# Output products in 32-row bands, decays from logarithms and exponentials, all stacking issued from SP

## The reference

```python
mag = np.sqrt(a_re * a_re + a_im * a_im)
scale = np.minimum(mag, 0.999) / (mag + 1e-06)
a_re_n, a_im_n = (a_re * scale, a_im * scale)      # 4 batches, 8 heads, 768 steps, 48 wide
for t in range(S):
    new_re = ar * S_re - ai * S_im
    new_im = ar * S_im + ai * S_re
    S_re, S_im = (new_re + kv, new_im)              # kv = k_t outer v_t
    y[:, :, t] = np.einsum('bhd,bhde->bhe', q[:, :, t], S_re)
x = y as [3072 tokens, 384]
h = x @ w_in;  g = h * clip(h + 3, 0, 6) / 6;              x = g @ w_out      # 384 -> 2048 -> 384
h = x @ w_in;  g = max(h, 0) + alpha * min(h, 0);          out = g @ w_out
```

## Time and profile before

| | us |
|---|---|
| three runs | 1082.05, 1083.62, 1083.95 |
| median | 1083.62 |
| the profiled execution | 1083.26 |
| its span, first to last instruction | 1081.5 |
| PE busy | 1009.7 (93%) |
| DVE busy | 703.4 (65%) |
| ACT busy | 487.5 (45%) |
| POOL busy | 305.8 (28%) |

### The profile page before, as it was taken

How to read it: one execution, slowest core, us unless ns; L and a number is a source line. 1 busy time by engine, 2 the same in 40 slices (tenths; PEclk the granted TensorE clock), 3 DMA queues, 4 the chain that set the end, 5 groups by cost and what they waited for, 6 DMA issues and landing times.

```text
span 1081.5 us, 16917 instructions
## 1 busy us (share of the span) xinstructions
PE 1009.7 (93%) x6354; PEld 1005.0 (93%) x6354; DVE 703.4 (65%) x1234; ACT 487.5 (45%) x814; POOL 305.8 (28%) x291
## 2 busy tenths in 40 slices
PE   0477789999999999999999999999999999999998
PEld 0477789999999999999999999999999999999997
DVE  4966999998998988889988234553433434343332
ACT  4644765676656666667664244331212212122221
POOL 3213421222222222222122233333333233333332
PEclk9968999999999999999999999999999999999999
DMA  5451233323233333232222070100101010101000
GB/s 182 132 147 30 67 95 99 94 67 88 68 77 102 87 87 89 67 89 67 70 74 74 13 277 1 45 24 22 45 1 44 1 45 1 44 1 45 1 22 23
DMA packets 77858, 70.47 MB, mean 65 GB/s; under 512 B 32592, under 2 KB 73552, under 8 KB 77392
## 3 DMA queue, kind: packets, MB, share of 16 engines
q1 hardware_dynamic: 68176, 61.07, 19.4%
q10 hardware_dynamic: 9600, 8.33, 2.9%
HBM read 40.90 MB, written 9.44 MB: 47 GB/s over the span
## 4 chain that ended last, share of the span: by engine, by line
PE 86%; DVE 7%; issue 2%; ACT 2%; SPq 1%; DMA 1%; ACTq 0%; DVEq 0%
PE op L995 12%; PE op L997 12%; PE op L996 12%; PE hp L997 12%; PE hp L995 12%; PE hp L996 12%; PE yp L980 5%; PE yp L983 4%; PE gp L990 2%; PE gp L959 2%; PE yp L959 2%; DVE t_inv L649 1%; PE tp L968 1%; DVE t_phase L665 1%; SPq L335 1%
## 5 line engine op out<-in xcount | busy, mean ns | idle before, releaser
L439 POOL TENSOR_TENSOR g_lo<-gated,g_hi 128x384 fp32r<-128x384 f32 x256 | 269.5, 1053 | 697.4 <-ACT g_hi L528 697.3
L528 ACT ACTIVATE g_hi<-gated 128x384 fp32r<-128x384 f32 x256 | 133.5, 522 | 357.5 <-DVE gated L761 291.4
L757 DVE TENSOR_SCALAR gate<-hp,alpha_sb 128x384 f32<-128x384 f32 x128 | 79.1, 618 | 230.5 <-PE hp L997 230.5
L995 PE MATMUL op<-g_hi,wb_hi 128*128 128x384 f32 x384 | 135.4, 353 | 2.3 <-POOL g_lo L439 2.3
L995 PE MATMUL hp<-x_hi,wa_hi 128*128 128x384 f32 x384 | 131.1, 341 | 6.1 <-DVE gated L747 6.1
L521 ACT ACTIVATE gate<-hp,half 128x384 f32<-128x384 f32 x128 | 73.7, 576 | 126.8 <-PE hp L997 115.0
L995 PE MATMUL op<-g_hi,wa_hi 128*128 128x384 f32 x384 | 129.9, 338 | 0.7 <-issue 0.7
L996 PE MATMUL op<-g_lo,wb_hi 128*128 128x384 f32 x384 | 130.0, 338 | 0.0
L997 PE MATMUL op<-g_hi,wb_lo 128*128 128x384 f32 x384 | 129.9, 338 | 0.0
L997 PE MATMUL op<-g_hi,wa_lo 128*128 128x384 f32 x384 | 129.8, 338 | 0.0
L997 PE MATMUL hp<-x_hi,w2i_lo 128*128 128x384 f32 x384 | 129.5, 337 | 0.0
(11 more groups left out here) (97 smaller groups left out, 1978.5 us busy)
## 6 DMA issues: line engine op xcount, KB each, us to landing
st<-prod SPq DMA_DIRECT2D x48, 145.1 KB, 3.1
st<-prod ACTq DMA_DIRECT2D x48, 145.1 KB, 2.8
a_sb<-a_in SPq DMA_DIRECT2D x24, 288.0 KB, 3.5
qk_sb<-qk_in SPq DMA_DIRECT2D x24, 288.0 KB, 3.5
v_pad<-v_in SPq DMA_DIRECT2D x24, 192.0 KB, 3.2
x<-out_sb SPq DMA_DIRECT2D x8, 576.0 KB, 2.8
x_raw<-x SPq DMA_DIRECT2D x8, 576.0 KB, 4.6
out<-out_sb SPq DMA_DIRECT2D x8, 576.0 KB, 3.1
```

Of the source, the lines that this page charges most:

```text
L439: pool.tensor_tensor(g_lo[:, at, :], gated[:, at * UT:(at + 1) * UT], g_hi[:, at, :].bitcast(F32), ALU.subtract).then_inc(glo_done, 1)
L528: act.activation(g_hi[:, at, :], gated[:, at * UT:(at + 1) * UT], ACT.Copy).then_inc(ghi_done, 1)
L757: dve.tensor_scalar(gate[:, at], hp[:, n % 2, 0:UT], 0.0, alpha_sb[:, m:m + 1], ALU.min, ALU.mult).then_inc(gate_done, 1)
L995: pe.matmul(acc, lhs[0], rhs[0], start=start, stop=False)
```

## The change

1. **Output products (PE).** Each quarter of 32 output rows is now a product of its own, with 32 columns of weights, written to one of the four 32-row quarters of `yp`. A band of 32 rows touches one head or two. The products go round the four quarters in turn: 16 with v, and 16 with the state, for each chunk, where 10 and 10 stood. The padding around v and the state shrinks from 176 to 80 columns for each head.
2. **Decays (ACT, DVE).** Square root, reciprocal and clamp are gone. ACT takes the logarithm of re² and of the squared magnitude in one instruction (L499), the magnitude as exp(0.5 log) (L502), 1/|re| as exp(-0.5 log) (L506), and 1e-6/(mag + 1e-6) by another logarithm and exponential (L508, L510). DVE corrects the inverse by a Newton step (`residue`, `refine`), and forms ratio and decay (`ratio`, `lost`, `decays`). L499 and L502 stand at position 2, behind `high`; L506 to L510 at position 3, behind `high`; before, the square root stood at position 1.
3. **Tables.** `angle` loads the table set `trig_and_small` explicitly, which serves arctangent and sine.
4. **Chunk ends.** The end decays are copied to `prod` by ACT (`copy_ends`, position 2, behind `high`) and not by DVE. SP waits for that before it stacks. The check for too small decays is moved to the end.
5. **Stacking.** All 12 DMAs of a chunk are issued by SP. The load of a goes from position 2 to position 4.

```diff
+def quarter(q, with_state):
+    for j, heads in bands(q):
+        parts = [(h, col, of_state) for of_state in ((False, True) if with_state else (False,)) for h, col in heads]
...
             def stack(c):
                 need(sp, y_ready, c - 1)
                 need(sp, state_ready, kept(c - 1))
+                sp.wait_ge(ends_set, c + 1)
                 sp.wait_ge(prod_done, 2 * c + 1)
...
-                for to, rows in high_stack(c, 1, HIGH_PARTS[:2]):
+                for to, rows in low_stack(c, 1) + high_stack(c, 1):
...
-            def magnitude(c):
-                act.wait_ge(m2_done, c + 1)
-                need(act, clip_done, c)
-                act.activation(flat(t_mag, 0), flat(t_sq, 0), ACT.Sqrt).then_inc(mag_set, 1)
+            def logs(c):
+                act.wait_ge(m2_done, c + 1)
+                need(act, inv_done, c)
+                act.activation(t_log[:, :, :, :], t_sq[:, :, :, :], ACT.Ln).then_inc(log_set, 1)
+                act.wait_ge(log_set, c + 1)
+                need(act, decay_done, c)
+                act.activation(flat(t_mag, 0), flat(t_log, 1), ACT.Exp, scale=0.5).then_inc(mag_set, 1)
+            def inverses(c):
+                need(act, ratio_done, c)
+                act.activation(flat(t_inv, 0), flat(t_log, 0), ACT.Exp, scale=-0.5).then_inc(inv_set, 1)
+                act.wait_ge(mag_set, c + 1)
+                act.activation(flat(t_eps, 0), flat(t_mag, 0), ACT.Ln, bias=tiny[:, 0:1]).then_inc(eps_set, 1)
+                act.wait_ge(eps_set, c + 1)
+                act.activation(flat(t_eps, 0), flat(t_eps, 0), ACT.Exp, bias=log_tiny[:, 0:1], scale=-1.0
+                               ).then_inc(part_set, 1)
...
-                dve.reciprocal(t_inv[:, 0, k, :], t_inv[:, 0, k, :]).then_inc(inv_done, 1)
...
+            def residue(c):
+            def refine(c):
+            def ratio(c):
+            def lost(c):
+            def decays(c):
...
+                for products in zip(*[quarter(q, not is_first(c)) for q in range(P // BAND)]):
+                    for q, (j, h, col, of_state, first, last) in enumerate(products):
+                        weights = (s_pad if of_state else v_pad)[:, col:col + BAND]
+                        mm = pe.matmul(yp3[q * BAND:(q + 1) * BAND, j, :], weights,
+                                       st[:, c % 2, h, 0, 0:CH] if of_state else scores[:, h, :], start=first, stop=last)
```

More of the change, by code:

```diff
@@ L262, in low_stack, with high_stack @@
                      prod[r * HD:(r + 1) * HD, x, :, :, :].rearrange("p k q t -> p k (q t)")) for r in range(2)]
[L264 removed]
+        def high_stack(c, x):
             return [(st[x * HD + d0:x * HD + d0 + rows, c % 2, h, :, :].rearrange("p q t -> p (q t)"),
[L266 removed]
+                     prod[p0:p0 + rows, x, k, :, :].rearrange("p q t -> p (q t)")) for p0, rows, k, h, d0 in HIGH_PARTS]
         def x_cols(c):
@@ L371, in _ @@
                         sp.dma_start(alpha_sb[:, :], alpha[:, :]).then_inc(alpha_landed, 16)
+                if pos == 4:
+                    c4 = chunk_at(s + 4)
+                    if c4 is not None and c4 >= 2:
+                        load_a(c4)
                 if n is not None and n % MT_FF == MT_FF - 1:
@@ L571, in _ @@
                     copy_k(c0, 0)
-                if pos == 1:
-                    if keeps:
-                        copy_k(c0, 1)
+                if pos == 1 and keeps:
+                    copy_k(c0, 1)
+                if pos == 2:
+                    if c1 is not None:
+                        copy_ends(c1)
                     if c2 is not None:
-                        magnitude(c2)
-                if pos == 2 and c1 is not None:
-                    stack(c1)
+                        logs(c2)
+                if pos == 3 and c2 is not None:
+                    inverses(c2)
                 if pos == 4 and c3 is not None:
@@ L975, in outputs @@
                     pe.wait_ge(state_ready, kept(c))
-                for j, heads in enumerate(tiles):
-                    for i, (h, row) in enumerate(heads):
-                        cols = slice(P + h * PADW - row, P + h * PADW - row + P)
-                        ends = i == len(heads) - 1
-                        mm = pe.matmul(yp3[:, j, :], v_pad[:, cols], scores[:, h, :], start=(i == 0),
-                                       stop=(is_first(c) and ends))
-                        if not is_first(c):
-                            mm = pe.matmul(yp3[:, j, :], s_pad[:, cols], st[:, c % 2, h, 0, 0:CH], start=False,
-                                           stop=ends)
+                for products in zip(*[quarter(q, not is_first(c)) for q in range(P // BAND)]):
[3 more added lines that the diff above has]
+                                       st[:, c % 2, h, 0, 0:CH] if of_state else scores[:, h, :], start=first, stop=last)
                 mm.then_inc(y_ready, 1)
```

178 lines of the change are left out of this document (86 added, 92 removed).

## The result

| | before | after |
|---|---|---|
| median, us | 1083.78 (4 runs, 1082.05 to 1084.64) | 1177.87 (4 runs, 1176.74 to 1181.12) |
| ratio after / before | | 1.0875, 95% interval 1.085 to 1.0901 |
| profiled span, us | 1081.5 | 1176.5 |

What follows compares the result with a forecast made beforehand. PE bounds the kernel, with ACT's serial list right behind; the change puts ACT's turn above PE. Span 1081.5 plus 88.8 for 20 turns, 12 ahead, 2.4 and -0.9 at the end gives 1183.8, forecast 1186 us, range 1160 to 1215.

Steps and rivals of the forecast that it cites:

- The reserve of 1.8: Five-item slots before the change: ACT's loop with DVE takes 22.2 us, PE needs 24.0, leaving 1.8 us.
- The turn of 28.0: ACT's list from A (end of `angle`) to the next A: 28.0 us for five items, 30.8 for six.
- The 20 turns: From A of chunk 3 to A of chunk 23: 567.1 us against 478.3 before, +88.8.
- DVE's saving worth nothing: DVE's dropped reciprocals, clip and wide products stand at positions 2 to 4, where DVE waits for ACT: no gain.
- Worth almost nothing until the last chunk: PE's faster outputs: idle 4 to 5 us a slot under the 28 us turn; gain 0.9 us at the last chunk.
- Outputs in 3.6 us by pairs: PE's 64 output records per chunk with state run in pairs: 3.6 us; one after another 7.1, four side by side 1.8.
- rival 4: ACT's gain stays under the reserve and PE stays the bound: 1064 us by pairs, 1026 four side by side; 5%.
- Rival 1: Output quarters queue on PE, outputs come too late for position 2's `high`: 0.8 to 3 us a slot, 1198 to 1231; 11%.
- SP: Twelve stacking issues take 8.7 us; scores can start 23.3 after A; hidden except at chunk 23, +2.4 us.
- The start: Chunks 0 to 2: +3 us each from ACT's list, +2.9 from extra issues, together +12; A of chunk 3 near 113.
- Rival 2: Clock falls as PE waits 4 to 5 of 28 us; half speed puts PE on the loop: above 1215; 4%.
- Rival 3: Logarithm and exponential share one loaded table set, three of four loads on ACT's turn go: 24.2 us turn, 1111; 5%.

Runs made afterwards that it cites:

- experiment 2: Kernel before with only the 32-row output products of the change, decays, ends and stacking as before; 1059.33 us (0.9761).
- 3: Kernel before with one useless table load a slot on ACT at position 3, behind `high`; 1089.96 us (1.005).
- experiment 4: Kernel before with three useless table loads a slot on ACT at position 3, behind `high`; 1142.54 us (1.0547).
- experiment 1: Changed kernel with the output products 128 columns wide again, all else as changed; 1185.6 us (1.0939).
- Experiment 5: Changed kernel with the table set holding both logarithm and exponential loaded by name ahead of L499; 1115.7 us (1.0298).
- 6: Kernel of experiment 5 with ACT's copy of the chunk ends moved ahead of `high` of position 2; 1089.88 us (1.0049).
- 9: Kernel of experiment 5 with logs and inverses at position 1, trigonometric load behind them, ends copied ahead of `high`, Newton step one position earlier; 1118.87 us (1.0332).
- 11: Changed kernel with only logs and inverses moved to position 1, five loads and the copy's place kept; 1209.77 us (1.1161).
- kernel 12: Kernel 9 with the chunk ends copied by DVE, as in the kernel before, and not by ACT; 1056.38 us (0.9753).
- kernel 8: Kernel of experiment 2 with the trigonometric table set loaded at the end of position 1, behind the square root; 1050.16 us (0.9689).
- experiment 7: Changed kernel with four of the twelve stacking DMAs back on ACT, behind the copy of the ends; 1253.74 us (1.1561).

## Why the prediction was right, point by point

- **The bound.** Read from ACT's and DVE's lists, not from the busy share of 45%: a loop of 22.2 us under PE's 24. Experiments 2, 3 and 4 show it from three sides: with PE relieved, turns stop at 22.45; a load of 1.28 costs 0.23; two more cost 2.42 of 2.57. The reserve of 1.8 "for each five-item slot" was too large: it holds for the turns of 24.0 us, is nothing at the turns to chunks 14 and 20, and is 0.8 in the mean of all slots (24.36 against 23.60). The forecast, with 5.8 us added, did not hang on it.
- **The turn of 28.0** measured 27.54 in the steady part (505.97 to 533.51 above), and six items 30.5 instead of 30.8. Term by term, predicted and measured from end to end: 12.0 and 11.95; copy 0.2 and 0.1; logs 3.9 and 4.0; position 3, 1.7 and 1.6; inverses 4.3 and 4.3; position 4, 1.7 and 1.6; squares and abs 1.2 and 1.14; gate 0.6 and 0.47; rest 2.4 and 2.38. The 0.46 too much is overlap: one activation starts some 0.1 us before the one ahead of it ends, and I counted most of them at full length. The prices taken for unknown functions held: logarithm of 768 columns 0.85 (0.83 taken), exponentials 0.51 to 0.53, with a bias tile 0.61.
- **The 20 turns**: 566.0 against 567.1. That is nearer than the terms, and luck: the 15 later turns took 6.6 us less than forecast, and the five early ones, to chunks 4 to 8, 5.5 more (27.7, 29.0, 24.3, 29.3 and 28.2; the two of four items were to take 26.3 each).
- **DVE's saving worth nothing, and PE's nearly nothing, in the steady part**: experiment 1 gave the same turn with wide outputs. For DVE it is read from its waits alone, 3.1 to 3.3 us twice a turn (183 us in all); no run gave it back its old work. "Worth almost nothing until the last chunk" was wrong for the first three chunks, by 7 us.
- **Outputs in 3.6 us by pairs** was wrong: 64 records take 1.97 us, 0.031 each against 0.11. The first and the second 32 of them differ by 0.89 us, where 20 wide ones differ by 2.23: a quarter for each record. So all four quarters run side by side, and the two records of one product don't hold the next quarter up. PE is off the path, so it cost the forecast under 2 us, at the last chunk; but rival 4 would have been priced by the wrong one of its two cases. Rival 1, outputs that come too late, did not come: in the slot shown the last output record ends at 513.77, and `high` waits for DVE until 517.39.
  The Trainium skill ("TensorEngine Tiling (Array Packing)", Theoretical Speedup) gives up to 4x for 32 columns; a whole output takes 4.62 us for 40 records before and 1.97 for 64 after, 3.8x less for each, so the trace agrees with it.
- **SP.** Twelve issues take 7.7 us and not 8.7: six on SP alone take 3.85, where the earlier trace rows had 4.33 with ACT issuing at the same time. Scores start 21.25 after A in chunk 23, not 23.3; at the end this showed as +0.4 instead of +2.4. The prediction took the 20.9 of before as the time of the stacking, but it was PE that came late there: in experiment 2, with the same stacking, scores of chunk 23 start 17.56 after A. The new stacking is 3.7 us slower than that, hidden under the turn.
- **The start** was +8.5 at A of chunk 3 instead of +12. The first chunk lost 2.8 (3 taken). Without the bands it would have been +15.7 (A of chunk 3 at 117.29 in experiment 1): the step was 4 too low for ACT's list and SP, and left out 7.2 that PE's short outputs gave back.
- **Rival 2, the clock**: the granted clock is 0.92 from 400 to 700 us, and falls to its lower level (1.2 GHz, half) for short stretches. From chunk 6 on, behind waits of 1.2 to 3.9 us the eight score records take between 1.16 and 2.08 us instead of 1.05; the length of the wait alone does not tell which. PE was off the loop: in the turn shown ACT does not wait for it from 517.39 on.
- **Rival 3, fewer loads**: the kernel has five loads a chunk, 121 in all, as the list of instructions told. Experiment 5 shows that the rival's mechanism is real. The Trainium skill ("ScalarE: Activation LUTs", Table sets: the hidden batching unit) counts one load for a logarithm and then an exponential; the trace agrees only for the kernel that loads the shared set by name. My 1111 for it was near (1115.7) by luck: the 20 turns took 507.4 us and not 496, since the second loop through the stacking held them, and the start cost 2.8 and not 8.
- **What I did not see**: that second loop. It decided experiments 5, 6, 9 and 11; the expectations of 5, 9 and 11 failed in the same way, each priced from the first loop, though 5 and 9 named the stacking as what could end later. In the forecast it cost nothing, since it was hidden under the longer one.
- **A sign that did not come**: ACT was to wait for PE nearly nowhere. In the turn shown it waits 1.64, 0.38 and 1.34 us for PE ahead of the `high` at 517.39 (all under DVE's work). The other signs came: one wait for `gated` at position 2, PE busy 85%, 121 loads; A of chunk 3 stood at 110.07 and not 113.

What stays open: whether kernel 12 with four issues back on ACT in the first slots, or kernel 8 with the Newton step in place of the reciprocals, is faster than 1050 us. Neither was tried.

## What to carry to other kernels

Two in-order engines that answer each other once a slot form a loop whose length no busy share shows: add up the list from one fixed instruction to its next, and compare the sum with the busiest engine's work per slot; the difference is the reserve, and an addition costs little up to it and nearly all of its length beyond (here 0.23 of 1.28 us, then 2.42 of 2.57). Take the reserve from every kind of slot, not from the one with the most work. Before moving work out of one loop, walk the others through its new place: here a copy of 0.2 us that starts a DMA queue was worth 62 us behind the wrong neighbours. Load by name one table set that serves all the functions of a stretch, at a place where the engine would wait anyway.

## What the runs showed of the chip that I had not expected

- Output products of 32 rows in four different quarters overlap: 64 records take 1.97 us and 32 take 1.08, where 40 and 20 records of 128 rows take 4.62 and 2.39, with the two parts of one product in the same quarter.
- DMA issues cost 0.64 us each on SP alone, and 0.81 on SP with 0.84 on ACT when both start at once (experiment 7).
- A DVE operation that meets POOL's `g_lo` can take 0.6 to 0.8 us longer, a 128x3 one as much as a 128x384 one: in the kernel after, POOL's starts at 511.24 and 529.59 fall beside these two, while the same lines take 0.17 and 0.55 at their shortest (source lines: shortest, median, longest ns).

```profile
511.60 0.79 DVE L714 TENSOR_SCALAR end_floor<-t_fb 128x3 f32<-128x3 f32 x1
...
529.81 1.36 DVE L675 TENSOR_TENSOR t_dt<-a_sb,t_inv 128x384 f32<-128x384 f32 x1
```

```profile
L714 DVE TENSOR_SCALAR end_floor<-t_fb x24: 169/794/958, 28.8 to 681.7; 128x3 f32<-128x3 f32 x24
...
L675 DVE TENSOR_TENSOR t_dt<-a_sb,t_inv x24: 550/1364/1379, 21.6 to 673.5; 128x384 f32<-128x384 f32 x24
```

  The trace of the kernel after bears it out for these two lines. The 18 of L714 that overlap a `g_lo` took 0.79 us or more, and each ended 0.02 to 0.03 us behind the end of that `g_lo`; the 6 others took 0.17. The 17 of L675 that overlap one took 1.35 or more and ended 0.41 to 0.42 behind it; the 7 others took 0.55. So they look held until `g_lo` is done. It does not hold for every operation: L681 started 0.25 us ahead of a `g_lo` 17 times and took 0.55. That POOL is the cause was not isolated by a run.
- A table load costs its 1.28 us also when nothing uses the set (experiment 4).
